# A fused recurrent-attention and two-layer feed-forward kernel: another beginning, and the second feed-forward's products in pairs

## What is computed

```python
for t in range(S):                       # B, H, S, D = 4, 8, 768, 48
    cur = np.einsum('bhd,bhe->bhde', u[None] * kt, vt)
    y[:, :, t] = np.einsum('bhd,bhde->bhe', rt, state + cur)
    state = wt[:, :, :, None] * state + np.einsum('bhd,bhe->bhde', kt, vt)
x = y as (3072 tokens, 384)
h = x @ w_in;  g = h * clip(h + 3, 0, 6) / 6;  x = g @ w_out     # w_in 384 x 2048, w_out 2048 x 384
h = x @ w_in2; g = h * sigmoid(h);             out = g @ w_out2
```

## Time and profile before

| | us |
|---|---|
| median of 3 runs | 936.35 (935.58 to 936.41) |
| the profiled execution | 933.82 |
| its span, first to last instruction | 932.0 |
| PE busy | 903.5 (97%) |
| DVE, ACT, POOL busy | 466.9, 319.8, 155.0 |
| mean granted TensorE clock | 0.980 of 2.4 GHz |

### The profile page before, as it was taken

One profiled execution on the slowest core, in us unless ns is written; L12 is line 12 of the kernel. 1 busy time (PEld: TensorE's weight loads), 2 busy tenths in 40 slices (PEclk: granted clock), 3 DMA queues, 4 the chain that ended last, 5 costly groups with the idle time before them and its releaser, 6 DMA issues.

```text
span 932.0 us, 15412 instructions
## 1 busy us (share of the span) xinstructions
PE 903.5 (97%) x5876; PEld 778.0 (83%) x5876; DVE 466.9 (50%) x692; ACT 319.8 (34%) x537; POOL 155.0 (17%) x154
## 2 busy tenths in 40 slices
PE   5589999999999999999999999999999999999998
PEld 4468888888888888888888799999899999989997
DVE  6866746665674666566445543333342333333332
ACT  2343333333333333333345532332332332332322
POOL 7453412322241332224000000000000000000000
PEclk7679999999999999999999999999999999999999
DMA  8452130213113021311203100000000000000000
GB/s 278 155 179 62 52 100 19 61 49 110 55 55 97 13 77 33 110 55 45 101 35 100 36 1 1 35 0 0 34 0 0 34 0 0 34 0 0 34 1 34
DMA packets 13367, 48.54 MB, mean 52 GB/s; under 512 B 1568, under 2 KB 2208, under 8 KB 13344
## 3 DMA queue, kind: packets, MB, share of 16 engines
q1 hardware_dynamic: 13344, 48.23, 16.2%
HBM read 43.50 MB, written 4.72 MB: 52 GB/s over the span
## 4 chain that ended last, share of the span: by engine, by line
PE 93%; DVE 2%; POOL 1%; DMA 1%; issue 1%; ACT 1%; SPq 0%; ACTq 0%; POOLq 0%; DVEq 0%
PE bank L682 14%; PE bank L683 14%; PE bank L684 14%; PE bank L711 7%; PE bank L713 7%; PE bank L712 7%; PE bank L699 7%; PE bank L701 7%; PE bank L700 7%; PE bank L747 2%; PE bank L778 2%; PE bank L783 1%; PE bank L760 1%; PE bank L735 1%; DVE w_lo L528 1%
## 5 line engine op out<-in xcount | busy, mean ns | idle before, releaser
L682 PE MATMUL bank<-x_hi,w_hi 128*128 (+1 forms) x576 | 228.1, 396 | 1.6 <-DVE x_lo L590 1.6
L683 PE MATMUL bank<-x_lo,w_hi 128*128 (+1 forms) x576 | 227.2, 394 | 0.0
L684 PE MATMUL bank<-x_hi,w_lo 128*128 (+1 forms) x576 | 227.1, 394 | 0.0
L397 ACT CAST g_hi<-g 128x512 fp32r<-128x512 f32 x192 | 119.3, 621 | 282.2 <-PE bank L713 144.2
L517 DVE TENSOR_TENSOR g<-g,bank 128x512 f32<-128x512 f32 x96 | 66.0, 688 | 243.6 <-ACT g L391 243.6
L524 DVE TENSOR_TENSOR g_lo<-g,g_hi 128x512 fp32r<-128x512 f32 x192 | 146.3, 762 | 0.9 <-ACT g_hi L397 0.9
L711 PE MATMUL bank<-w_hi,g_hi 128*128 128x384 f32 x384 | 129.6, 337 | 1.2 <-ACT x L443 1.2
L713 PE MATMUL bank<-w_hi,g_lo 128*128 128x384 f32 x384 | 129.6, 337 | 0.0
L682 PEld LDWEIGHTS bank<-x_hi,w_hi 128*128 128x128 f32 x576 | 109.0, 189 | 24.1 <-DVE x_lo L590 2.1
L712 PE MATMUL bank<-w_lo,g_hi 128*128 128x384 f32 x384 | 129.0, 336 | 0.0
L684 PEld LDWEIGHTS bank<-x_hi,w_lo 128*128 128x128 f32 x576 | 108.8, 189 | 23.4
(11 more groups left out here) (91 smaller groups left out, 809.6 us busy)
## 6 DMA issues: line engine op xcount, KB each, us to landing
unit_in<-rkv_tm SPq DMA_DIRECT2D x23, 576.0 KB, 5.8
unit_in<-rk_fm SPq DMA_DIRECT2D x23, 448.0 KB, 3.8
x<-w SPq DMA_DIRECT2D x8, 768.0 KB, 5.1
unit_in<-w SPq DMA_DIRECT2D x8, 768.0 KB, 4.3
unit_in<-w_fm SPq DMA_DIRECT2D x23, 226.2 KB, 5.0
out<-tmp SPq DMA_DIRECT2D x5, 768.0 KB, 3.3
out<-tmp SPq DMA_DIRECT2D x4, 192.0 KB, 2.0
x<-rkv_tm SPq DMA_DIRECT2D x1, 576.0 KB, 11.6
```

Source lines behind the costliest of these rows:

```text
L397: nc.scalar.copy(g_hi[:, p, :], g[:, p, :]).then_inc(ghi_done, 1)
L682: nc.tensor.matmul(h_ps[j % 2][:, :], wh, xh, start=k == 0, stop=False)
L683: nc.tensor.matmul(h_ps[j % 2][:, :], wh, xl, start=False, stop=False)
L684: last = nc.tensor.matmul(h_ps[j % 2][:, :], wl, xh, start=False, stop=k == KT - 1)
```

## The change

- **Loads.** Each first unit has its own place (`firsts`), so none waits for another; only v is loaded in token order (192 KB instead of 576 KB). u also comes as columns, by two strided loads of 4-byte elements. Chunks 0 and 1 come between the units, the rest as their buffers come free, and the loads of the next step's units are written out between them.
- **Decays and own term of the first units.** Keys and queries are multiplied by their decays on DVE (`first_decays`). GpSimd makes one product r times k a unit (`first_products`); TensorE multiplies it with the u columns (`first_own`, 4 matmuls of 2 columns); ACT copies the 8 sums out, and also copies the state (which DVE did, line 585).
- **Order.** The pieces of the first units are written out by hand on each engine. TensorE gets 45 more transposes of the identity in between (`spin_matmuls`: 8, 10, 3, 12, 2, 10).
- **Weights.** Only chunks 0 and 1 are split before the first layer. Chunks 2 to 7 are split in the first step of layer 1, which is written out of its loop, at the slots of `WHI_SLOTS` (ACT) and `WLO_SLOTS` (DVE). GpSimd splits none.
- **Layer 2.** `hidden` and `sums2` are taken in pairs of tiles.

```diff
-        PRO_SPLITS = {1: [0], 2: [1], 3: [2, 3], 4: [4], 5: [5]}
...
-        TILE_SPLITS = {0: [6], 1: [7]}
...
+        WHI_SLOTS = {1: 2, 2: 3, 4: 4, 5: 5, 7: 6, 8: 7}
+        WLO_SLOTS = {1: 2, 3: 3, 5: 4, 6: 5, 8: 6, 9: 7}
...
+                if b == 0:
+                    sp.wait_ge(u_zeroed, 1)
+                    for q in range(2):
+                        sp.dma_start(u_cols[ODD * q:ODD * q + D, :].rearrange("p (i q) -> p i q", q=2)[:, :, q],
+                                     u_row.rearrange("o (i q d) -> (o q) d i", i=PAIRS, q=2)[q], allow_slow_non_contiguous=True).then_inc(u_loaded, 16)
+                sp.dma_start(v, rkv_tm[b, :, 2 * DM:3 * DM]).then_inc(first_v_loaded[b], 16)
...
+            def first_decays(b):
+                rk, w, v = firsts[b]
+                scan(b, w, first_w_loaded[b], 16)
+                forward(b, w)
+                dve.wait_ge(prod_done, b + 1)
+                nc.vector.tensor_tensor(rk[:, 1], rk[:, 1], segs(back)[:, :, 1:SEG], ALU.mult).then_inc(kt_done, 1)
+                dve.wait_ge(fwd_done, b + 1)
+                nc.vector.tensor_tensor(rk[:, 0], rk[:, 0], segs(fwd[:, :])[:, :, 0:C], ALU.mult).then_inc(rt_done, 1)
...
+            def first_own(b):
+                rk, w, v = firsts[b]
+                pe.wait_ge(prod_done, b + 1)
+                if b == 0:
+                    pe.wait_ge(u_loaded, 32)
+                else:
+                    pe.wait_ge(kt_kept, b)
+                    pe.wait_ge(own_done, b)
+                for i in range(PAIRS):
+                    at = PAIRS * KROWS + 2 * i
+                    last = nc.tensor.matmul(first_keys[:, at:at + 2], rk_prod[:, i, :], u_cols[:, 2 * i:2 * i + 2], start=True, stop=True)
+                last.then_inc(own_full, 1)
+                pe.wait_ge(own_done, b + 1)
...
             with pe.Fori(0, STEPS - 1) as c:
-                for j in range(2, FT + 2):
+                for j in range(2, FT + 2, 2):
                     if j == FT:
                         pe.wait_ge(x2lo_done, KT * (c + 2))
-                    hidden(FT * (STEPS + c) + j, j, c + j // FT, CHUNKS)
+                    for t in (j, j + 1):
+                        hidden(FT * (STEPS + c) + t, t, c + t // FT, CHUNKS)
...
-                    sums2(FT * (STEPS + c) + j - 2, j - 2)
+                    for t in (j - 2, j - 1):
+                        sums2(FT * (STEPS + c) + t, t)
```

More of the change, by code:

```diff
@@ L340, in own_diagonal @@
             def own_diagonal(b, a, c):
[L341 removed]
+                nc.gpsimd.affine_select(out=a_sb, in_=own.unsqueeze(2).to_broadcast([P, H, C]),
                                         compare_op=ALU.is_equal, fill=0.0, base=0, pattern=[[0, H], [1, C]],
@@ new lines, in first_state, with xhi @@
+            def first_state(b):
+                act.wait_ge(outer_full, b + 1)
+                act.wait_ge(sums_v, 1)
+                outer = first_outer[:, 0:PAIRS * D].rearrange("p (i e) -> p i e", i=PAIRS)
+                for q in range(2):
+                    rows = slice(ODD * q, ODD * q + D)
+                    nc.scalar.copy(state[b][rows, :, D * q:D * q + D], outer[rows, :, :]).then_inc(added, 1)
+            def xhi(b, a, step, x_bank):
+                act.wait_ge(y_full, a + 1)
+                nc.scalar.copy(x_view(x_hi, step, b), x_bank[:, 0:DM].rearrange("p (k t) -> p k t", k=KT)).then_inc(xhi_done, 1)
@@ new lines, in first_mask, with attention @@
+            def first_mask(b):
+                dve.wait_ge(diag_done, b + 1)
+                for q in range(2):
+                    dve.wait_ge(scores_full, 2 * b + q + 1)
+                    late_scores(q, a_sets[b % 2], first_scores[b % 2][q])
+            p_last = segs(back)[:, :, 0:1]
+            def attention(slot, c):
+                for b, k in run_pieces(slot):
+                    a = B * (c + 1) + b
+                    banks = run_banks[b]
+                    rk, w, tm = units[b % 2]
+                    if k == SCAN:
+                        dve.wait_ge(masked, 2 * a)
+                        scan(a, w, w_loaded[b % 2], 16 * taken(b, c))
@@ new lines, in region, with from_state, from_scores @@
+            def region(x_bank, n):
+                return x_bank[Q * (n % 4):Q * (n % 4) + Q, n // 4 * P:n // 4 * P + C]
+            def from_state(b, rk, x_bank):
+                for n in range(REGIONS):
+                    i, e = n // 3, n % 3 * Q
+                    last = nc.tensor.matmul(region(x_bank, n), state[b][0:KROWS, i, e:e + Q], rk[:, 0, i, :], start=n < 4, stop=False)
+                last.then_inc(queries_read, 1)
+            def from_scores(b, a, v, scores, x_bank, first):
+                pe.wait_ge(v_mid_done, a + 1)
+                for n in range(REGIONS):
+                    i, e = n // 3, n % 3
+                    values = v_mid[b % 2][:, i, 0, :] if e == 1 else v[:, n * Q:n * Q + Q]
+                    last = nc.tensor.matmul(region(x_bank, n), values, scores[:, e // 2 * PAIRS + i, :], start=first and n < 4, stop=False)
+                if first:
+                    last.then_inc(queries_read, 1)
+                for n in range(1, REGIONS, 3):
+                    i = n // 3
+                    last = nc.tensor.matmul(region(x_bank, n), v_mid[b % 2][:, i, 1, :], scores[:, PAIRS + i, :], start=False, stop=True)
+                last.then_inc(y_full, 1)
@@ L791, in _ @@
-            pe.wait_ge(consts, 3)
-            for _ in range(WARM_UP):
-                nc.tensor.transpose(bank[7][:, 0:P], ident[:, :], ident[:, :])
-            pe.wait_ge(sums_v, 1)
-            for slot in range(PRO_SLOTS):
-                attention(slot, PRO, 0, None)
+                        raw_scores(a, rk, banks)
+                    if k == OUTER:
+                        pe.wait_ge(masked, 2 * a + 2)
+                        pe.wait_ge(tm_loaded[b % 2], 16 * taken(b, c))
+                        outer(a, tm[:, 2, :], banks[2])
```

509 lines of the change are left out of this document (289 added, 220 removed).

## The result

| | before | after |
|---|---|---|
| median, us | 936.38 (935.58 to 936.55, 4 runs) | **919.68** (918.57 to 920.81, 4 runs) |
| ratio, 95% interval | | 0.9823 [0.9806, 0.984] |
| the profiled execution, its span | 933.82, 932.0 | 920.81, 919.1 |
| first hidden | 47.44 | 37.71 |
| from there to the hidden of tile 16 | 86.52 | 83.93 |

The change takes 16.7 us off the median; I had said 21.4 (914.95 us, the forecast's own range 912 to 918, the whole range 910.5 to 923.5): the result lies in the whole range and outside the forecast's own. The two profiled spans differ by 12.9 only, because before's profiled execution was 2.6 us under its median and after's is 1.1 over: 12.9 + 2.6 + 1.1 = 16.6. The lower four rows of the table split the 12.9: 9.7 + 2.6 + 1.4 - 0.8. In which stretch those other 2.6 us lie in before's other executions, no profile shows.

The account below looks back on a forecast made before the run. TensorE, busy 97% of the span, was taken as the bound. Terms 13.5 + 7.5 - 2.1 + 3.0 - 0.5 = 21.4 us gave 936.35 - 21.4 = 914.95 us; own range 912 to 918, whole range 910.5 to 923.5.

Parts of the forecast that it names:

- The beginning: Before layer 1: the first hidden matmul starts at 33.9 us instead of 47.4, 13.5 us gained.
- I walk TensorE's own order at full clock: Beginning: first transposes to 7.3 us, four units 15.7, added transposes 10.2, one wait 0.7, together 33.9 us.
- Rival 1: Beginning: the clock falls for one or two stretches; 3.4 us cost 1.7, 6.8 cost 3.4; 916.7 to 918.4; chance 0.17.
- Rival 2: Clock down through the beginning: from 12.2 us all doubles but overlapping waits; first hidden about 44, time 925; chance 0.10.
- The first tiles: Layer 1's first step: all 7.5 us lost before the first visit come back; new waits lose 2.1.
- My two places: Step 0 of layer 1: waits at sums of tiles 1 (0.6) and 0 (0.1); unit 5's scores 1.2, next visit 0.2.
- up to 2.5 us each: Step 0 of layer 1: bound on each w_lo on DVE in slots 5 and 6, making the backlog grow by 2.3.
- Pairs with the tail: Layer 2: 48 pairs save 3.0 us; a longer wait at the sums of tile 14 loses 0.5.
- my two terms: Layer 2, saved per pair of slots: one hidden 0.04 us and one sums2 0.026, given as 0.063 a pair.
- Covers that held: Beginning: u loads, taken at 1.0 us, hide behind the first transposes; DVE stays just behind TensorE's order.
- Rivals 3 and 4: 3: layer 2's pairs give nothing, 918.0, chance 0.12. 4: layer 1's chunk conversions become the bound, 939.6, chance 0.03.
- before's distance of 2.5 us: Whole kernel: the median was 2.5 us above the profiled execution, and this distance was kept for the forecast.

Follow-up runs that it names:

- after_again: The changed kernel run once more, with no edit; 918.65 us, ratio 0.9814 to the kernel before.
- begin_only: The changed kernel with layer 2 tile by tile as before, leaving the new beginning alone; 920.57 us, ratio 0.9837 to the kernel before.
- pool_decays: The changed kernel with the decays' products of the first four units back on GpSimd; 919.43 us, ratio 0.9822 to the kernel before.
- early_chunks: The changed kernel with chunks 2 and 3 split before the first tile's gate; 923.55 us, ratio 0.9865 to the kernel before.
- visit_slots: The changed kernel with the low parts of chunks 3, 5 and 7 and one high part a slot later, unit 6 loaded before chunk 7; 918.36 us.
- tail_order: The changed kernel with g_lo of tile 14 before the gate of tile 15 at layer 2's end; 917.72 us, ratio 0.9803 to the kernel before.
- padded_end: The kernel best with eight one-column memsets on DVE behind its last g_lo; 914.53 us, ratio 0.9767 to the kernel before.
- best: The changed kernel with own sums in their own bank, tail_order's edit, low parts in slots without a scan, and visit_slots' load order; 916.36 us.
- pairs_only: The kernel before with only layer 2 taken in pairs of tiles; 935.01 us, ratio 0.9991 to the kernel before.
- best_pool: The kernel best with the decays' products of the first four units on GpSimd; 917.16 us, ratio 0.9795 to the kernel before.

## Why the prediction came out as it did

Direction, place and whole range were right; the gain was 4.7 us smaller than forecast and lies outside the forecast's own range, to which I gave 0.58. Against the profiled spans (12.9 us gained) the terms are off by 8.5 us, of which 3.7 come back because before's profiled execution was faster than its median and after's slower. That part is luck.

- **The beginning, 13.5 forecast, 9.7 measured (11.4 and 12.7 in after_again and begin_only).** The step "I walk TensorE's own order at full clock" failed. With the kernel's order unchanged, after_again, begin_only and after have 6.8, 3.4 and 13.7 us at half clock and start layer 1 at 36.04, 34.77 and 37.71. These, pool_decays (36.14) and early_chunks (36.79 at 10.2) lie within 0.3 us of a line, 34.0 us plus 0.27 for each us at half clock (visit_slots, 36.27 at 6.8, is 0.4 over it). Its end at none is my 33.9, but by luck, since errors cancel: 45 transposes cost 5.1 at full pace and not 10.2, while own sums with their copy cost 1.22 a unit and not 0.85, the own sums and DVE's products of units 0 and 1 wait for GpSimd's product (DVE stands idle 1.09 and 1.10 us for it in after, a wait that my walk did not have), and DVE's scans beside that product take 1.7 to 2.3 us instead of 1.23. Rival 1 is what came in these runs, in after with twice the most half clock that it had (13.7 against 6.8 us). Its price of half a us for each us at half clock was too high; likely because TensorE's waits for GpSimd and DVE shrink while its own work is slower (2.1 us of them in units 0 and 1 of after_again, 0.9 in after). Rival 2's "all doubles" does not give its 44 as it is worded (21.7 us doubled without the waits end near 53); 44 comes out only because the transposes were priced at the half pace already. The half pace up to 22 us of tail_order started layer 1 at 37.74. The sentence from TensorE: Matmul & The Clock Gate (Part 1) in the Trainium skill, that the moment varies from run to run, agrees with these traces, which vary more than the 500 ns that the page gives: the pace first doubled between 5.7 and 8.8 us in twelve profiles and at 22 us in two, and the first recorded fall came at 9.14, 14.10 and 14.99 us in the three. I had read it and still gave the full clock the higher chance.
- **The first tiles, 7.5 regained and 2.1 lost again: 5.4 forecast, 2.6 measured.** The 7.5 came back; from the first hidden to tile 16 it would be 79.0 us without waits (86.52 - 7.5), and 83.93 is 4.9 more. So the new waits were 4.9, not 2.1. My two places were right: about 1.4 us at the sums of tiles 0 and 1 against 0.7, some 1.7 at the scores of units 5 and 6 against 1.4. (The recorded waits are 0.60, 1.00 and 0.56 of this; the rest is what passes beyond the pace around them, against the same matmuls of before.) The missing one is the sums of tile 3, 1.6 us with what trails it, and it failed on the bound "up to 2.5 us each" for a w_lo beside GpSimd. The rows had nothing dearer than 2.29, and I had not put GpSimd's order beside DVE's in slot 3.
- **Pairs with the tail, 3.0 - 0.5 = 2.5 forecast, 1.4 measured.** The mechanism and its size were right: 0.07 us a pair (my two terms, 0.04 and 0.026, add up to 0.066 and not 0.063). Of 48 x 0.067 = 3.2 us are given back 0.67 us at the end (forecast 0.5; tail_order brings it back) and 0.22 us in each of five steps, where the second hidden of the pair with the split of x2 starts late, for which the walk had no term: TensorE of after, the end of one hidden and the beginning of the next, 0.35 instead of 0.23 us apart:

```profile
545.36 0.40 PE L774 MATMUL bank<-x_hi,w_lo 128*128 x1
545.71 0.49 PE L772 MATMUL bank<-x_hi,w_hi 128*128 x1
546.04 0.39 PE L773 MATMUL bank<-x_lo,w_hi 128*128 x1
```

- **The end, nothing forecast, 0.8 lost.** DVE's first of the last two copies starts late, the stores queue up behind it and land later. padded_end removes it with eight instructions ahead of the copy, so it is no wait of the change's; it goes with the packet of instructions that moves among the stores.
- **Covers that held:** the u columns landed 4.0 us after their issue, at 6.36 us the later one in after, ahead of the own sums, which waited for GpSimd's product until 7.6. That DVE stays behind TensorE's order from unit 2 on fits pool_decays: with 1.4 us a unit taken off DVE the start did not move. In units 0 and 1 it does not hold in every profile (after_again waits 0.71 and 0.83 us for DVE's products). Rivals 3 and 4 did not come; 4's backlog exists (chunk 3), at 1.1 us.
- **The median.** I kept before's distance of 2.5 us between profiled execution and median for the new kernel. It was not there: the profiled execution lies 1.1 us over the median in after, 2.7 under it in begin_only and 2.8 over it in tail_order.

## What to carry to other kernels

When a walk through an engine's order is to give a start time, take the durations at the clock that the stretch had before (read from the instructions' pace, since the clock column prints 1.00 where it has no record), and give the better clock a chance, not the sum. When conversions are moved under other work, put the two engines that disturb each other side by side by order, slot by slot: the same 128x1536 subtraction cost 1.75 or 4.67 us depending on what stood beside it, and moving it a slot did not lengthen the kernel. A hand-over (copy out, wait, go on) on the bounding engine is worth a bank of its own if one is idle, here 1.4 to 1.6 us at the first hidden, in three profiles.

## What was not expected of the hardware

- A DVE subtraction of 1.75 us took 4.67 us beside four GpSimd instructions in a row, of which the first three kept their own times of 1.0 to 1.2 us and the fourth went from 1.20 to 2.26; in visit_slots a g_lo of 0.69 took 3.02 beside the same four. At other places GpSimd's product took 2.2 us instead of 1.2 and DVE's scan beside it 1.72 instead of 1.23. Which of the two yields was not settled.
- Every profile starts at half pace (transposes 0.213 us apart, later 0.109), and this lasts until 5.7 to 8.8 us, in tail_order and best until 22. The clock record begins just there in all 14, as far as matmuls lie around it, so that a mean clock of 1.000 (tail_order, best) belongs to kernels with 14 us at half pace.
- The last but one copy on DVE starts 0.81 us behind the start of the matmul that it waits for in all nine profiles with the changed kernel's DVE program at that place, and 0.44 us behind in the five others (before, pairs_only, pool_decays, best_pool, padded_end). Eight instructions more or fewer ahead of it remove the 0.37 us. In the nine, and only there, an 8 KB packet of instructions moves among the last stores, so that the instructions arrive late is likely. Not shown is how the packet holds up the copy, which starts late 0.7 us or more before the packet moves.
